# Attention, low-rank mixing and phase mixing on one core: the first batch's phases and weights in another order, Q and K in three buffers

## The chip, the cores and the metric

The kernel runs on one core of a Trainium2 chip. The metric is the device time of one launch in microseconds (us), the median of a few runs; lower is better.

## What is computed

The reference, cut to what matters. There are 4 batches, 8 heads, 768 tokens and a head size of 48, so a row has D = 384 features.

```python
mag = np.sqrt(a_re * a_re + a_im * a_im)
scale = np.minimum(mag, 0.999) / (mag + 1e-06)
a_re_n, a_im_n = (a_re * scale, a_im * scale)
for t in range(S):                       # the state is complex, k v^T is added to its real part
    new_re = ar * S_re - ai * S_im
    new_im = ar * S_im + ai * S_re
    S_re, S_im = (new_re + kv, new_im)
    y[:, :, t] = np.einsum('bhd,bhde->bhe', q[:, :, t], S_re)
# y as x of shape (batch, seq, 384)
h = xt @ U @ V                           # over the tokens, rank 32
u = x + h.transpose(0, 2, 1)
x = u + np.maximum(u @ w_ch1, 0.0) @ w_ch2
theta = x @ w_theta
y = np.einsum('ts,bsd->btd', w_tok_r, x * cos(theta)) + np.einsum('ts,bsd->btd', w_tok_i, x * sin(theta))
u = x + y
out = u + np.maximum(u @ w_ch, 0.0)
```

## The kernel before

The recurrence over tokens is done as chunked attention. A batch is C = 6 chunks of P = 128 tokens. For every token and feature the kernel takes the logarithm of the magnitude of `a` and its angle, sums both over the tokens (the sums of the angle, in turns, are the phases), and multiplies Q and K by a decay factor (`scaled`) and then by the sine and the cosine of the phase (`turned`, r = 0 and 1), which gives the tensor `QKz`. DMAs turn its features into rows (`to_rows`, two DMAs for each r, since features are spread over heads in a wide and a fine group). On these rows PE computes the scores of the chunk (`scores`), DVE masks them (`mask_scores`), and PE adds masked scores times V and Q times the state (`values`). The state goes from chunk to chunk: PE transposes K (`key_columns`), ACT copies it (`keys_to_sbuf`), PE multiplies K and V (`keys_values`), ACT copies the product (L735), PE transposes it (`turn_state`), and DVE adds and decays the state (`next_state`, L1085 to L1091). After the chunks come the low-rank mixing (`rank`, `u_rows`, `u_mixed`), the two channel products (`up`, `down`), `theta`, the token products (`mix`) and the last channel product (`channels`). Those products take their operands in two parts: a rounded part that ACT makes (`round_piece` for the weights, L867) and the rest, which POOL makes by subtraction (`split`, L534). Weights come in 15 pieces: 0 to 11 for the two channel products, 12 to 14 for the last two matrices.

Five programs, one an engine, run beside each other and meet in semaphores; what stands in a program is done in that order. The order is written out by hand. SP issues nearly all DMAs. From batch 1 on, the phases and decays of the next batch are computed during the channel products of the batch before. Batch 0 has its own way (functions named `first_...`): ACT and DVE make logarithms and tangents chunk by chunk, PE sums the decays (`first_sums`), ACT takes six arctangents (`first_angle`, L640), and PE sums the angles of a chunk over its tokens by a product with a triangular matrix and adds the carry of the chunk before (`first_turns`). A negative real part needs half a turn more; `phasor[:, c, 0, :]` holds 0 or 0.5 for that, and PE adds it with three products of its own, beside the three for the angle, which are multiplied by `tri_turn` (the triangle over pi). DVE then takes the carry of the chunk and the fraction of the phase (`first_phase`, L995 to L1006), ACT sine and cosine (`first_sin_cos`, L646 to L649).

In batch 0 the order around the change is: five phases on PE and DVE, then the scores of chunk 0, then phase 5 on PE (`first_turns(C - 1)` in `attention`) and on DVE behind the masks of chunk 0. Between phases DVE scales and turns Q and K of chunks 0 and 1. ACT issues the r = 1 half of chunk 0's rows itself (`first_rows`). ACT rounds two pieces behind each chunk of batch 0, POOL splits eight of them, then squares the next batch's `a`, and splits the last four among the work for batch 1. Q and K come through two buffers, `qk_in`, which are the first 4 D columns of `stream`; `load_qk(b, c)` waits until chunk c - 2 is turned. SP loads Q and K of chunk c + 3 and V of chunk c + 2 ahead of the rows of chunk c + 2.

## Time and profile before

| | |
|---|---|
| median of 3 runs | 774.71 us (773.43 to 777.81) |
| the profiled execution's own time | 773.47 us |
| its span, from the first to the last instruction | 771.7 us |
| PE, matmul | 731.8 us busy (95%) |
| DVE | 499.9 us busy (65%) |
| ACT | 403.8 us busy (52%) |
| POOL | 223.6 us busy (29%) |
| mean granted clock of PE | 0.989 of full speed |
| chain that ended last, by engine | PE 81%, DVE 7%, ACT 4%, DMA 4% |

Busy time is the union of an engine's instructions. In the span of batch 0 up to 98.6 us the chain goes through all engines; behind it PE is nearly always busy. A timeline row gives start and length in us, then how many instructions of one kind it stands for, and in brackets how long the engine was idle before it and what ended that.

### The profile page before, as it was taken

To read this page: it belongs to the slowest core of one execution; us is meant where nothing else is said; L and a number is where in the kernel's file an instruction comes from. 1 tells how busy PE (TensorE), PEld (TensorE's weight loads), DVE (VectorE), ACT (ScalarE), POOL (GpSimd) and SP (SyncE) were. 2 spreads that over 40 slices of the span, in tenths; PEclk is the share of its full clock that TensorE was granted. 3 is DMA by queue.
4 is the path that set the end of the run, shared out by engine and by line. 5 is a ranking of instruction groups with operands and counts; after the bars stand their busy time and mean duration, and the time that the engine had idled before them with its cause. 6 is when DMAs were issued, how large, how long until landed. Compare 5 with 4: busy or idle time off the path is not lost.

```text
span 771.7 us, 13433 instructions
## 1 busy us (share of the span) xinstructions
PE 731.8 (95%) x5118; PEld 704.2 (91%) x5118; DVE 499.9 (65%) x905; ACT 403.8 (52%) x875; POOL 223.6 (29%) x175
## 2 busy tenths in 40 slices
PE   3588999999999999999999999999999999999998
PEld 3578799999999879999999879999999979999998
DVE  7759488798468657696558758597448832224534
ACT  7847456755365447664464537574464621223531
POOL 0006663533520063323430053232530010113350
PEclk9889999999999999999999999999999999999999
DMA  9566620100257750010246860010136940000121
GB/s 301 169 184 180 196 87 1 41 1 2 82 145 213 209 174 1 4 39 1 62 133 184 218 205 21 2 42 1 50 96 185 254 135 23 2 1 0 42 62 62
DMA packets 42735, 73.48 MB, mean 95 GB/s; under 512 B 8784, under 2 KB 23376, under 8 KB 42672
## 3 DMA queue, kind: packets, MB, share of 16 engines
q1 hardware_dynamic: 42384, 72.23, 31.9%
q8 instruction: 41, 0.67, 0.4%
q10 hardware_dynamic: 288, 0.39, 0.2%
q14 instruction: 22, 0.18, 0.1%
HBM read 48.96 MB, written 4.72 MB: 70 GB/s over the span
## 4 chain that ended last, share of the span: by engine, by line
PE 81%; DVE 7%; ACT 4%; DMA 4%; issue 2%; SPq 1%; DVEq 0%; ACTq 0%
PE bank L1302 78%; DMA stream<-stream 2%; DMA region<-stream 1%; PE bank L1507 1%; DVE stream L1041 1%; DVE logr L915 1%; DVE logr L911 1%; PE bank L1418 1%; PE bank L1343 1%; PE bank L1375 1%; SPq L357 1%; DVE phasor L904 1%; DVE stream L1055 0%; SPq L358 0%; DVE ST L1072 0%
## 5 line engine op out<-in xcount | busy, mean ns | idle before, releaser
L1302 PE MATMUL bank<-uT,w_sb 128*128 128x384 f32 x864 | 166.5, 339 | 0.0
L1302 PE MATMUL bank<-hT,w_sb 128*128 128x384 f32 x864 | 165.0, 336 | 0.0
L1302 PE MATMUL bank<-tok,z 128*128 128x384 f32 x864 | 158.7, 337 | 0.6 <-issue 0.2
L1302 PEld LDWEIGHTS bank<-uT,w_sb 128*128 128x128 f32 x864 | 151.6, 190 | 1.8 <-ACT uT L756 1.2
L1302 PEld LDWEIGHTS bank<-hT,w_sb 128*128 128x128 f32 x864 | 151.1, 188 | 0.3 <-DVE hT L1200 0.3
L1302 PEld LDWEIGHTS bank<-tok,z 128*128 128x128 f32 x864 | 149.3, 188 | 1.7 <-POOL tok L539 1.7
L1200 DVE SCALAR_TENSOR_TENSOR hT<-bank,hT 128x384 fp32r<-128x384 f32 x96 | 52.8, 550 | 68.1 <-ACT hT L748 67.7
L748 ACT ACTIVATE hT<-bank 128x384 fp32r<-128x384 f32 x96 | 46.4, 484 | 75.4 <-PE bank L1302 75.3
L539 POOL TENSOR_TENSOR tok<-tok_low,tok 128x768 fp32r<-128x768 f32 x20 | 38.2, 1909 | 86.7 <-ACT tok L778 86.7
L547 POOL TENSOR_TENSOR x_sb<-uT 128x384 f32<-128x384 f32 x24 | 25.1, 1077 | 104.1 <-DVE uT L1194 71.1
L514 POOL TENSOR_TENSOR logr<-stream 128x384 f32<-128x384 f32 x18 | 15.1, 841 | 102.1 <-DMA stream<-in_a 102.1
L534 POOL TENSOR_TENSOR w_sb<-w_raw,w_sb 128x768 fp32r<-128x768 f32 x12 | 26.1, 2189 | 63.7 <-ACT w_sb L867 63.7
L553 POOL TENSOR_TENSOR xs<-x_sb,xs 128x384 fp32r<-128x384 f32 x24 | 27.7, 1173 | 54.5 <-ACT xs L765 54.5
L1302 PE MATMUL bank<-tc_sb,xs 128*128 128x384 f32 x216 | 41.4, 335 | 0.0
L1072 DVE TENSOR_TENSOR ST<-bank,tri 128x512 f32<-128x512 f32 x48 | 32.5, 687 | 13.2 <-PE bank L1302 12.9
L1302 PE MATMUL bank<-xs,tc_sb 128*128 128x384 f32 x216 | 38.9, 337 | 0.0
L519 POOL TENSOR_TENSOR phasor<-stream,phasor 128x384 f32<-128x384 f32 x18 | 18.8, 1046 | 68.6 <-ACT phasor L665 68.6
L1302 PEld LDWEIGHTS bank<-tc_sb,xs 128*128 128x128 f32 x216 | 37.9, 188 | 0.0
L1302 PEld LDWEIGHTS bank<-xs,tc_sb 128*128 128x128 f32 x216 | 37.4, 188 | 0.0
L539 POOL TENSOR_TENSOR tok<-scale,tok 128x768 fp32r<-128x768 f32 x16 | 29.4, 1848 | 25.9 <-ACT tok L778 25.9
L1302 PE MATMUL bank<-region 96*128 96x128 f32 x256 | 33.3, 286 | 3.6 <-DMA region<-stream 3.6
L1302 PEld LDWEIGHTS bank<-region 96*128 96x128 f32 x256 | 31.7, 200 | 4.1 <-DMA region<-stream 4.0
(183 smaller groups left out, 1309.5 us busy)
## 6 DMA issues: line engine op xcount, KB each, us to landing
stream<-in_qk SPq DMA_DIRECT2D x24, 384.0 KB, 3.9
tok_low<-in_w_tok SPq DMA_DIRECT2D x20, 384.0 KB, 3.5
stream<-in_a SPq DMA_DIRECT2D x19, 384.0 KB, 3.8
scale<-in_w_tok SPq DMA_DIRECT2D x16, 384.0 KB, 4.2
w_raw<-in_w SPq DMA_DIRECT2D x12, 384.0 KB, 7.8
region<-qk SPq DMA_DIRECT2D x16, 256.0 KB, 3.6
region<-stream SPq DMA_DIRECT2D x15, 256.0 KB, 3.2
stream<-in_v SPq DMA_DIRECT2D x16, 192.0 KB, 4.3
```

What stands on the lines that cost most here:

```text
L357: sp.dma_start(to[wide, :, :, :], QKz[c % 2][:, r, 0:2, :, :]).then_inc(s_rows_in[c % 3].sem, 16)
L514: ins = g.tensor_tensor(to, part, part, ALU.mult)
L519: g.tensor_tensor(phasor[:, c, 1, :], a_part(b, c, 1), phasor[:, c, 1, :], ALU.mult)\
L534: g.tensor_tensor(part[1], raw, part[0].bitcast(F32), ALU.subtract).then_inc(s_split.sem, 1)
L539: g.tensor_tensor(tok[:, m % 4, 1, :], tok_raw(m)[1], tok[:, m % 4, 0, :].bitcast(F32), ALU.subtract)\
L547: g.tensor_tensor(x_sb[:, n, :], uT[:, 0, kd, :].bitcast(F32), uT[:, 1, kd, :].bitcast(F32), ALU.add)\
L553: g.tensor_tensor(xs[0][:, 1, n % KD, :], x_sb[:, n, :], xs[0][:, 0, n % KD, :].bitcast(F32), ALU.subtract)\
L748: a.activation(hT[:, n % 3, 0, :], hidden_bank[n % 3][:, 0:N2], ACT.Relu).then_inc(s_hid_hi.sem, 1)
L904: d.tensor_tensor(mag, mag, qk[:, c * D:(c + 1) * D], ALU.add).then_inc(s_den.sem, 1)
L1072: d.tensor_tensor(ST[:, 4 * i:4 * i + 4, :], heads(score_bank[i][:, :]), tri[:, :].unsqueeze(1).broadcast_to([P, 4, P]), ALU.mult)\
L1200: d.scalar_tensor_tensor(hT[:, n % 3, 1, :], hidden_bank[n % 3][:, 0:N2], 0.0, hT[:, n % 3, 0, :].bitcast(F32), ALU.max, ALU.subtract)\
L1302: return t.matmul(o, lhsT, rhs, start=start, stop=stop, is_transpose=turned)
```

## The change

It has four parts.

1. Batch 0's sign term leaves PE. A new DVE operation a chunk (`first_turn`) multiplies the angle by 1/pi and adds the half turn, in place; `first_turns` on PE has three products with `tri` instead of six, and waits for that operation; `tri_turn` is gone.
2. All six phases stand ahead of the first scores, on PE and on DVE. `key_columns(0, 0)` comes after three phases, not four. V's split stands behind the phases; the scaling of chunk 1 behind phase 2.
3. Weight pieces 0 to 3 are rounded on ACT one by one between the first sines and cosines, 4 to 9 behind the sixth, 10 and 11 behind chunks 0 and 1. POOL splits all twelve in a row ahead of the next batch's squares. Pieces 12 to 14 are loaded during chunk 2. ACT issues its half of chunk 0's rows before the third sine, not after.
4. Q and K have a third buffer, `qk_third`; `load_qk(b, c)` waits for chunk c - 3. SP issues the rows of chunk c + 2 first, then Q and K of chunk c + 4, then V of chunk c + 2. Chunk 2 of the next batch is loaded in the middle of the batch before.

```diff
-        qk_in = [stream[:, at * D:(at + 2) * D].rearrange("p (i j t) -> p i j t", i=G, j=2) for at in (0, 2)]
+        qk_third = sb("qk_third", [P, 2 * D])
+        qk_in = [at.rearrange("p (i j t) -> p i j t", i=G, j=2)
+                 for at in (stream[:, 0:2 * D], stream[:, 2 * D:4 * D], qk_third[:, :])]
...
-        EARLY = 2 * PIECES - 4
+        EARLY = 2 * PIECES
...
             def load_qk(b, c):
-                if c >= 2:
-                    sp.wait_ge(s_Q.sem, s_Q.at(b, c - 1))
+                if c >= 3:
+                    sp.wait_ge(s_Q.sem, s_Q.at(b, c - 2))
...
                 for c in range(C - 1):
-                    if c + 3 < C and (c >= 1 or b == 0):
-                        load_qk(b, c + 3)
+                    if c + 2 < C:
+                        to_rows(b, c + 2)
+                    if c + 4 < C:
+                        load_qk(b, c + 4)
                     if c >= 1 and c + 2 < C:
                         load_v(b, c + 2)
-                    if c + 2 < C:
-                        to_rows(b, c + 2)
...
+                    if b == 0 and c == 2:
+                        for n in range(2 * PIECES, STAGED):
+                            load_piece(n)
...
                     sp.wait_ge(s_quot.sem, s_quot.at(b_next, C))
+                    load_qk(b_next, 2)
...
             to_rows(0, 0)
-            load_qk(0, 2)
             to_rows(0, 1)
+            load_qk(0, 3)
             gains_to_rows(0)
-            for n in range(2 * PIECES, STAGED):
-                load_piece(n)
...
-                    if b == 1 and c < 3:
-                        split(EARLY + 1 + c)
...
-                if b == 0:
-                    split(EARLY)
...
                     attention(b, c)
-                    if b == 0:
-                        round_piece(2 * c)
-                        round_piece(2 * c + 1)
+                    if b == 0 and c < 2:
+                        round_piece(2 * PIECES - 2 + c)
...
+            round_piece(0)
             for c in range(C):
+                if c == G - 1:
+                    first_rows()
                 if c == G:
-                    first_rows()
                     keys_to_sbuf(0, 0)
                 first_sin_cos(c)
+                if c < G:
+                    round_piece(c + 1)
+            for n in range(G + 1, 2 * PIECES - 2):
+                round_piece(n)
...
+            def first_turn(c):
+
+                angle_c = phasor[:, c, 1, :]
+                dve.wait_ge(s_atan.sem, c + 1)
+                d.scalar_tensor_tensor(angle_c, angle_c, 1 / math.pi, phasor[:, c, 0, :], ALU.mult, ALU.add)\
+                    .then_inc(s_first_turn.sem, 1)
...
-                    if b == c == 0:
-                        first_phase(C - 1)
...
             def first_turns(c):
-                pe.wait_ge(s_atan.sem, c + 1)
+                pe.wait_ge(s_first_turn.sem, c + 1)
...
-                    mm(to, phasor[:, c, 1, at], tri_turn[:, :], start=i == 0, stop=False)
-                    ins = mm(to, phasor[:, c, 0, at], tri[:, :], start=False, stop=c == 0 and i == G - 1)
+                    ins = mm(to, phasor[:, c, 1, at], tri[:, :], start=i == 0, stop=c == 0 and i == G - 1)
...
-                if b == c == 0:
-                    first_turns(C - 1)
...
-            for c in range(G + 1):
+            for c in range(G):
                 first_turns(c)
             key_columns(0, 0)
-            first_turns(G + 1)
+            for c in range(G, C):
+                first_turns(c)
```

**DVE, from the first scaling to the first masks.** L1041 (L1051 in the change) is `scaled`, L995 to L1006 (L1005 to L1016) a phase, L1055 (L1065) `turned`, L1172 and L1174 (L1180 and L1182) V's split, L1072 (L1082) the masks. Before, from the first products of chunk 0 on:

```order
L1055 TENSOR_TENSOR stream<-stream,phasor 128x768 x2
L995 COPY carry<-bank 128x3
L1004 TENSOR_SCALAR phasor<-bank 128x384
L1006 TENSOR_TENSOR phasor<-bank,phasor 128x384
L1055 TENSOR_TENSOR qk<-stream,phasor 128x768 x2
```

The change:

```order
L999 SCALAR_TENSOR_TENSOR phasor<-phasor 128x384 x2
L1065 TENSOR_TENSOR stream<-stream,phasor 128x768 x2
L1005 COPY carry<-bank 128x3
L1014 TENSOR_SCALAR phasor<-bank 128x384
L1016 TENSOR_TENSOR phasor<-bank,phasor 128x384
L1051 TENSOR_TENSOR stream<-stream,first_scale 128x768
L1005 COPY carry<-bank 128x3
L1014 TENSOR_SCALAR phasor<-bank 128x384
L1016 TENSOR_TENSOR phasor<-bank,phasor 128x384
L1065 TENSOR_TENSOR qk<-stream,phasor 128x768 x2
```

The last two of the six sign additions (L999) stand ahead of chunk 0's products, and the scaling of chunk 1 and one more phase between these and chunk 1's.

**ACT, from the arctangents to chunk 0.** L640 (L639) are the arctangents, the three lines from L646 (L645) a sine and cosine, L655 and L656 (L654 and L655) the DMAs of `first_rows`, L867 (L865) a rounding, L735 (L734) the copy of the K-V product. Before, around the sixth sine:

```order
L646 ACTIVATE phasor<-phasor 128x384
L648 ACTIVATE phasor<-phasor,half_pi 128x384
L649 ACTIVATE phasor<-phasor 128x384
L735 ACTIVATE tA<-bank 112x384
L742 ACTIVATE region<-bank 128x512
L867 ACTIVATE w_sb<-w_raw 128x768 x2
```

The change:

```order
L645 ACTIVATE phasor<-phasor 128x384
L647 ACTIVATE phasor<-phasor,half_pi 128x384
L648 ACTIVATE phasor<-phasor 128x384
L865 ACTIVATE w_sb<-w_raw 128x768 x6
L734 ACTIVATE tA<-bank 112x384
L741 ACTIVATE region<-bank 128x512
L865 ACTIVATE w_sb<-w_raw 128x768
```

Six roundings now stand between the sixth sine and the copy of the K-V product.

**SP, chunks 1 and 2 of batch 1.** L357 and L358 (L359 and L360) are `to_rows`, L334 (L336) `load_qk`, L341 (L343) `load_v`, L392 (L394) `store`. Before, from the end of chunk 3's rows to chunk 4's:

```order
L358 DMA region<-qk 16x8x256
L392 DMA out<-tB 128x384 [waits s_out]
L392 DMA out<-tC 128x384 [waits s_out]
L334 DMA stream<-in_qk 128x768 [waits s_Q]
L341 DMA stream<-in_v 128x384 [waits s_yt]
L357 DMA stream<-stream 32x4x512 [waits s_Q,s_yt]
```

The change:

```order
L360 DMA region<-qk 16x8x256
L336 DMA qk_third<-in_qk 128x768 [waits s_Q]
L343 DMA stream<-in_v 128x384 [waits s_yt]
L394 DMA out<-tB 128x384 [waits s_out]
L394 DMA out<-tC 128x384 [waits s_out]
L359 DMA stream<-stream 32x4x512 [waits s_Q,s_yt]
```

The V transfer in this piece is that of chunk 3 instead of chunk 4; chunk 4's now stands behind chunk 4's rows.

## Rows read from the trace of the kernel before

**Rows 1.** Windows: stretch, busy us (count) of PE, PEld, DVE, ACT, POOL; clock, DMA share, GB/s.

```profile
98.60:237.40 138.80, 137.79 (x793) 136.34 (x793) 105.20 (x186) 82.00 (x173) 58.12 (x42) 0.99 0.17 52
```

**Rows 2.** Timeline of PE, first batch: start, length, engine, line, operation, count [idle].

```profile
37.18 1.21 PE L1302 MATMUL bank<-carry,ident 128*128 128x128 f32 x6
...
48.57 3.78 PE L1302 MATMUL bank<-region 96*128 96x128 f32 x16 [3.27 <-DMA region<-stream]
```

**Rows 3.** Timeline of DVE, first batch, same columns.

```profile
34.87 0.16 DVE L995 COPY carry<-bank 128x3 f32<-128x3 f32 x1 [0.53 <-PE bank L1302]
...
35.52 0.56 DVE L1006 TENSOR_TENSOR phasor<-bank,phasor 128x384 f32<-128x384 f32 x1
...
39.56 1.81 DVE L1055 TENSOR_TENSOR stream<-stream,phasor 128x768 f32<-128x768 f32 x2
...
50.69 0.69 DVE L1072 TENSOR_TENSOR ST<-bank,tri 128x512 f32<-128x512 f32 x1 [4.13 <-PE bank L1302]
...
56.80 0.95 DVE L1041 TENSOR_TENSOR stream<-stream,first_scale 128x768 f32<-128x768 f32 x1
```

**Rows 4.** Timeline of ACT, first batch; ACTq is a DMA that ACT issues.

```profile
32.57 2.59 ACT L640 ACTIVATE phasor<-phasor 128x384 f32<-128x384 f32 x6
...
43.83 0.61 ACTq L656 DMA_DIRECT2D region<-stream  x1
...
58.41 0.47 ACT L735 ACTIVATE tA<-bank 112x384 f32<-112x384 f32 x1
...
59.25 1.57 ACT L867 ACTIVATE w_sb<-w_raw 128x768 fp32r<-128x768 f32 x2
```

**Rows 5.** Windows: the stretch of the first scores, columns as in rows 1.

```profile
48.50:52.20 3.70, 3.63 (x17) 3.63 (x18) 0.69 (x1) 0.15 (x1) 0.00 (x0) 0.50 0.69 149
```

**Rows 6.** Lengths (ns, min/median/max) of two lines, and timeline of POOL and DVE.

```profile
L534 POOL TENSOR_TENSOR w_sb<-w_raw,w_sb x12: 1812/2169/2772, 60.2 to 122.0; 128x768 fp32r<-128x768 f32 x12
...
L1091 DVE TENSOR_TENSOR state<-state_sum,gain_rows x20: 553/555/1604, 60.2 to 621.8; 96x384 f32<-96x384 f32 x20
...
66.38 2.21 POOL L534 TENSOR_TENSOR w_sb<-w_raw,w_sb 128x768 fp32r<-128x768 f32 x1 [2.15 <-ACT w_sb L867]
...
66.38 4.95 POOL L534 TENSOR_TENSOR w_sb<-w_raw,w_sb 128x768 fp32r<-128x768 f32 x2 [2.15 <-ACT w_sb L867]
...
65.09 1.83 DVE L1055 TENSOR_TENSOR qk<-stream,phasor 128x768 f32<-128x768 f32 x2
...
67.41 1.60 DVE L1091 TENSOR_TENSOR state<-state_sum,gain_rows 96x384 f32<-96x384 f32 x1
```

**Rows 7.** Timeline of POOL and DVE: three scans beside a square, and alone.

```profile
108.85 0.94 POOL L514 TENSOR_TENSOR logr<-stream 128x384 f32<-128x384 f32 x1
...
109.14 2.15 DVE L915 TENSOR_TENSOR_SCAN logr<-logr,qk 128x128 f32<-128x128 f32 x3
...
129.16 1.06 DVE L915 TENSOR_TENSOR_SCAN logr<-logr,qk 128x128 f32<-128x128 f32 x3
```

**Rows 8.** Timeline of DVE: masks of chunks 1 and 4, then two chunks of batch 1.

```profile
61.10 0.69 DVE L1072 TENSOR_TENSOR ST<-bank,tri 128x512 f32<-128x512 f32 x1 [0.34 <-PE bank L1302]
...
83.10 1.27 DVE L1072 TENSOR_TENSOR ST<-bank,tri 128x512 f32<-128x512 f32 x2
...
249.12 0.69 DVE L1072 TENSOR_TENSOR ST<-bank,tri 128x512 f32<-128x512 f32 x1 [0.16 <-PE bank L1302]
...
255.06 0.69 DVE L1072 TENSOR_TENSOR ST<-bank,tri 128x512 f32<-128x512 f32 x1 [0.23 <-PE bank L1302]
```

**Rows 9.** Timeline of PE in batches 1 and 2, and one window (DMA share second last).

```profile
260.76 2.05 PE L1302 MATMUL bank<-stream 96*128 96x128 f32 x16 [0.69 <-DMA stream<-stream]
...
425.49 2.05 PE L1302 MATMUL bank<-region 96*128 96x128 f32 x16 [0.33 <-DMA region<-stream]
...
438.67 2.05 PE L1302 MATMUL bank<-stream 96*128 96x128 f32 x16 [1.03 <-DMA stream<-stream]
...
250.00:252.00 2.00, 2.00 (x39) 1.86 (x39) 1.70 (x3) 1.70 (x5) 0.00 (x0) 1.00 1.10 220
```

39 lines of the change are left out of this document (22 added, 17 removed).

## The prediction

> **What bounds the kernel now.** I read the windows first. From 98.6 to 237.4 us PE is busy for 137.8 of 138.8 us [rows 1]: products of the first batch's second half and of the mixing leave nothing to win, and splits that run there on POOL cost nothing. What the change can touch is the first batch up to 98.6 us and the attention chunks of batches 1 to 3.
>
> The timelines of the first batch come next. PE waits 3.27 us for the turned rows of chunk 0 [rows 2]; after that it runs its first 16 score passes in 3.78 us, where the same 16 take 2.05 us later [rows 2, 9], because the granted clock stands at 0.50, the lower of its two levels, 1.2 GHz [rows 5]. Last comes phase 5, behind the scores on PE; DVE can scale Q and K of chunk 2 only at 56.80, and ACT copies the first K-V product only at 58.41 [rows 3, 4]. From then to the mask of chunk 4 the chunks follow in (83.10 - 61.10) / 3 = 7.3 us, where batch 1 needs 5.94 [rows 8]. The difference is POOL. A split has 1.81 us of its own, and DVE's state update, 0.55 of its own, took 1.60 while a split ran [rows 6]. The reader is to see that both never work at once if DVE reads two operands from SBUF. Nor does DVE keep its turn: three scans, 1.06 us alone, took 2.15 because POOL's second square went in between them [rows 7]. POOL's first split of the pair at 66.38 took 2.21, so it really began about 66.78, 0.14 before the end of the product that it met [rows 6].
>
> In batches 1 to 3 PE waits only for rows that DMA turns round: 0.69 us in batch 1 and again in batch 3, of which one row is shown, 1.03 in batch 2, and 0.33 at chunk 2 of batch 2; the DMA engines' busy share is 1.10 there [rows 9].
>
> **The change, part by part.** The sum goes against the profiled execution, 773.47 us (span 771.7, 1.8 around it); its difference is then put on the median, 774.71. About 0.5%, 3.9 us, is what a measurement can tell from no change.
>
> *Sign on DVE.* PE loses 3 of 6 products per phase; DVE gets six additions of 0.55 us (its 384-wide two-operand length [rows 3]). The first one stands on the path: PE starts 0.6 us later and needs some 0.7 less, so phase 0 ends where it did, at 35.9 or so (36.08 before). PE ran slowly then (three carries 1.21 us [rows 2]), so phase 1 ends near 38.3.
>
> *Rounding early.* Arctangents end at 35.16 [rows 4]. Rounding is 0.79 us a piece, a sine and cosine about 1.5 (three of ACT's 0.43 steps and its own wait [rows 4]). Pieces 0, 1, 2 are then rounded by 35.9, 38.3 and 40.6, and each starts a split of 1.8 us. The fifth sign addition starts at 38.2, the split goes in behind it, the sixth addition waits until 40.3, and the third split lands before or between the two products of chunk 0. These end near 44.2; without POOL 41.1, before 41.37 [rows 3]. ACT's half of the turned rows, issued at 43.83 before [rows 4], goes out at about 44.9 and lands near 48.2, helped by an emptier queue: no gain.
>
> *All phases first.* DVE: phase 2 to 45.3 (1.2 us a phase [rows 3]), scaling of chunk 1 to 46.2, phase 3, which needs PE's six transposes, its turns and its carries, to 47.6, the two products of chunk 1 with split 3 between them to 50.9, phase 4 to 52.1, PE's carries 1.2 more, phase 5 to 53.3, V's split, a cast of 0.55 and a 768-wide difference of 0.95, to 54.8. The two masks end near 56.5, so chunk 2 is scaled at the same time as before (56.80 [rows 3]). ACT ends its last sine at 54.9, then rounds six pieces, 4.7 us, and comes to the K-V copy at 59.6; before 58.41. So the named idle time is used, but it is not idle any more: the phases have taken PE's and DVE's.
>
> *Splits in the chunks.* Eight splits are still to come from 55.8 on, POOL having a backlog. A turn of a 768-wide operation and a split lasts 0.95 + 1.82 less two overlaps of 0.13, 2.51 us; with the state update 2.11. A chunk has three of the first and one of the second: 9.6 us. The mask of chunk 1 comes at 65.4, of chunk 2 at 75.0, and then, POOL being done, two steps of 5.94 bring that of chunk 4 to 86.9: 3.8 us later than before. This is the upper end. The lower: DVE keeps the port through neighbouring products, two holds a chunk as now. Then chunk 0's products end at 42.5, the mask of chunk 1 comes near 60.1, and 22.0 us later, at the old pace, chunk 4's at 82.1: 1.0 us earlier. The scans [rows 7] speak for the upper end. Against it stands POOL's second split of the pair at 66.38: the pair took 4.95, so the second began at about 69.5, when the state update, done at 69.01, and the first mask had both passed it [rows 6]. I take the middle, **+1.4 us**. That ACT no longer rounds two pieces just ahead of the last copy of x is worth **-0.1** at most, taken as that.
>
> The Trainium skill, SBUF — State Buffer, section "SBUF: two separate sides", calls the pair of ports that DVE and GpSimd share an exclusive lock held for a whole instruction, and puts GpSimd's release at DVE's end plus about 115 ns. The lock agrees with the 1.60 us; the delay does not agree with a start 0.14 us ahead of that end [rows 6]. By the page eight turns would be 0.25 us longer each, 2.0 us in all, and the sum 775.8 instead of 773.8.
>
> *Three buffers, rows first.* The same bytes go out between the turned rows of chunk 3 and those of chunk 4, except V of chunk 4, 192 KB, which now follows: at 220 GB/s [rows 9] 0.85 us. Of the waits 0.69, 1.03 and 0.69 this takes 0.69, 0.85, 0.69, **-2.2 us**; the 0.33 stays. Bounds 0 (the total queue is as full) and -2.7 (all of them). V of chunk 4 must then land within the 7 us or so until PE's K-V products of that chunk; if this cover is gone, they wait. In the first batch the three last weight pieces now go out ahead of chunk 5's rows instead of beside the first ones: 1.15 MB, up to 1 us, within the range.
>
> *Splits taken out of the second half:* nothing, PE covers them [rows 1].
>
> Sum: 774.71 + 1.4 - 0.1 - 2.2 = **773.8 us**, no change that can be told.
>
> **Rivals.**
> - *DVE keeps its turn* (lower end above, -1.0, and all of -2.3): 771.4. For it: the passing over at 68 us. Against: the scans.
> - *POOL never meets DVE on the path.* DVE waited 4.13 us before the first mask [rows 3], so holds may fall there. Without any, chunk 0's products end at 41.1, chunk 2 is scaled at 51.4, the K-V copy comes at 55.3, the mask of chunk 1 at 58.0, that of chunk 4 at 58.0 + 3 x 5.94 = 75.8, 7.3 earlier: 774.71 - 7.3 - 2.3 = 765.1. Against it stands that ACT releases splits exactly while DVE has its two-operand work.
> - *Slower: the clock falls again.* With 9.6 us chunks PE, which has 5.94 of work, waits 3.6 us for the masks of chunks 1 and 2. The one wait of 3.27 us before the first scores was followed by 0.50 for 3.7 us [rows 2, 5], which costs half of that, 1.85. It decides once a wait reaches about that length. Two such and the upper end: 774.71 + 3.8 + 3.7 - 2.3 = 779.9.
> - *The reordering does nothing:* the engines stay full and the waits stay: 776.0.
> - *POOL gets the port later than I read*, which is what the page's figure above would mean: 775.8, worked out from eight turns of 0.25 us.
>
> **How the numbers follow.** Forecast 0.42; DVE keeps its turn 0.20; no holds on the path 0.16; clock falls 0.12; reordering does nothing 0.06; later port 0.04. Faster by over 0.5% (below 770.8): all of the third case, half of the second, a little of the first, 0.30. Slower (above 778.6): 0.12. The rest 0.58. The range goes from 766.0, which leaves out the better half of the third case, to 779.0, which leaves out the worse half of the fourth.
>
> **What would show it.** In the profile of the changed kernel: the first splits start at 36 us and the sixth sign addition or the first product of Q lasts 2 us or more; chunk 0's products end at 43.5 to 44.5; the K-V copy on ACT comes later than 58.4; in the next two chunks the products of Q are stretched to more than 2 us each, and the chunks last over 8 us; chunks 3 and 4 come at the pace of 5.9; PE's waits for turned rows in batches 1 to 3 shrink to about 0.5 us in all; the 98.6 to 237.4 us stretch keeps its length of 138.8. Wrong would be: products of Q at their own 0.95 us throughout (third case), a clock below 1 in the chunks (fourth), or the masks of chunk 4 earlier than 80 us.

## The result and the profile after

The changed kernel takes 780.55 us, the median of 14 runs (777.71 to 783.18), against 773.61 for the kernel before in the same session: a ratio of 1.0081 (95% 1.0066 to 1.0096), so it is slower by 0.8%. Its profiled execution took 781.37 us with a span of 779.6. In the code of after the masks are L1082 (L1072 before), the scaling L1051, the products L1065, the state update L1101, PE's products L1317 (L1302), a split L535 (L534), a rounding L865 (L867) and the copy of the K-V product L734 (L735); other kernels differ from these by a few lines. A product here is DVE's turning of Q and K, L1065, and a hold is the time that a DVE operation waits for a split that is under way.

First the timeline of DVE in the first batch, columns as in [rows 2].

```profile
37.00 1.71 DVE L999 SCALAR_TENSOR_TENSOR phasor<-phasor 128x384 f32<-128x384 f32 x1
...
39.75 2.45 DVE L999 SCALAR_TENSOR_TENSOR phasor<-phasor 128x384 f32<-128x384 f32 x2
42.12 3.42 DVE L1065 TENSOR_TENSOR stream<-stream,phasor 128x768 f32<-128x768 f32 x2
...
50.24 2.61 DVE L1065 TENSOR_TENSOR qk<-stream,phasor 128x768 f32<-128x768 f32 x2
...
56.64 1.29 DVE L1082 TENSOR_TENSOR ST<-bank,tri 128x512 f32<-128x512 f32 x2
...
57.85 0.95 DVE L1051 TENSOR_TENSOR qk_third<-qk_third,first_scale 128x768 f32<-128x768 f32 x1
...
58.83 2.45 DVE L1065 TENSOR_TENSOR stream<-qk_third,phasor 128x768 f32<-128x768 f32 x1
...
64.34 1.52 DVE L1101 TENSOR_TENSOR state<-state_sum,gain_rows 96x384 f32<-96x384 f32 x1
65.90 0.69 DVE L1082 TENSOR_TENSOR ST<-bank,tri 128x512 f32<-128x512 f32 x1
...
67.83 2.31 DVE L1051 TENSOR_TENSOR stream<-stream,first_scale 128x768 f32<-128x768 f32 x1
70.17 4.96 DVE L1065 TENSOR_TENSOR qk<-stream,phasor 128x768 f32<-128x768 f32 x2
...
77.13 1.27 DVE L1082 TENSOR_TENSOR ST<-bank,tri 128x512 f32<-128x512 f32 x2
```

A fourth sign addition of 1.71 us in place of 0.55, a pair of products of 3.42 in place of 1.81 [rows 3], a pair of 4.96: every DVE operation with two operands in SBUF that meets a split under way waits for it. The first masks, at 50.69 before [rows 3], come at 56.64; those of chunk 1, at 61.10 [rows 8], at 65.90; those of chunk 2 at 77.13, where the kernel before had them at 68.9.

POOL in the same stretch. The first row is the first of the four splits ahead of the scores. The last row is all eight splits that stand in a row behind them, the three ahead of it the first of these, the second with the third, and the third with the fourth, so that they start at 57.88, 60.43 and 62.92:

```profile
36.48 1.81 POOL L535 TENSOR_TENSOR w_sb<-w_raw,w_sb 128x768 fp32r<-128x768 f32 x1 [34.10 <-ACT w_sb L865]
...
57.88 2.59 POOL L535 TENSOR_TENSOR w_sb<-w_raw,w_sb 128x768 fp32r<-128x768 f32 x1 [6.71 <-ACT w_sb L865]
...
60.43 5.02 POOL L535 TENSOR_TENSOR w_sb<-w_raw,w_sb 128x768 fp32r<-128x768 f32 x2
...
62.92 4.62 POOL L535 TENSOR_TENSOR w_sb<-w_raw,w_sb 128x768 fp32r<-128x768 f32 x2
...
57.88 18.92 POOL L535 TENSOR_TENSOR w_sb<-w_raw,w_sb 128x768 fp32r<-128x768 f32 x8 [6.71 <-ACT w_sb L865]
```

ACT behind its last sine, and PE, where the bracket says how long it was idle and for what:

```profile
56.97 4.49 ACT L865 ACTIVATE w_sb<-w_raw 128x768 fp32r<-128x768 f32 x6
61.37 0.47 ACT L734 ACTIVATE tA<-bank 112x384 f32<-112x384 f32 x1
```

```profile
53.74 1.95 PE L1317 MATMUL bank<-region 96*128 96x128 f32 x16
...
61.89 0.98 PE L1389 MATMUL bank<-ident,tA 112*96 112x112 f32 x4 [3.26 <-ACT tA L734]
...
77.95 0.67 PE L1317 MATMUL bank<-ST,tD 128*48 128x128 f32 x4 [3.65 <-DVE ST L1082]
```

The copy of the K-V sums stands behind six roundings and comes at 61.37 (58.41 before [rows 4]); PE waits 3.26 us for it and 3.65 us for the masks of chunk 2. Windows of PE around these two waits (the clock is third from the end):

```profile
60.00:64.00 4.00, 2.11 (x11) 2.11 (x12) 4.00 (x3) 3.50 (x7) 4.00 (x3) 0.50 0.34 98
...
68.00:74.00 6.00, 6.00 (x86) 5.67 (x82) 5.97 (x3) 3.60 (x9) 6.00 (x3) 1.00 0.07 26
...
80.00:86.00 6.00, 6.00 (x48) 5.49 (x46) 3.29 (x6) 1.98 (x5) 0.00 (x0) 0.69 0.78 199
```

Each wait is followed by a stretch at 1.2 GHz; the last window, 0.69, holds a part of the second one. What went well shows too: the first 16 score passes took 1.95 us at the full clock, where they took 3.78 before [rows 2]. A phase's products now stand right ahead of them, in place of the wait of 3.27 us.

Where the 7.9 us between the two profiled spans lie: the channel products of batch 0 start at 107.1 in place of 98.6 us, which is 8.5; the attention of batches 1 to 3, from first mask to channel products, gives back 0.47 and 0.88 and loses 0.41; the rest of the layers gives 2.6 back in batch 0 and loses 1.6 and 1.4 in batches 1 and 2. Pieces of that last size come and go between profiles of kernels with the same work there, as the section on the hardware tells, so they are not put down to the change. The waits of PE for turned rows in batches 1 to 3 [rows 9] are down to 0.2 us, but PE now waits for V, here in batch 2, and 1.3 us in batch 3:

```profile
435.33 0.87 PE L1317 MATMUL bank<-qk,tD 128*48 128x96 f32 x16 [0.99 <-DMA tD<-in_v]
```

### The profile page after: what moved, and what is told of

Same layout as the page of the kernel before. It is cut to its first block, busy times and chain, and to the rows that moved or that the text cites. A ratio compares the mean times of both kernels' runs of the same rounds, so it can differ in the third digit from the quotient of the medians.

```text
span 779.6 us, 13366 instructions
## 1 busy us (share of the span) xinstructions
PE 735.4 (94%) x5082; PEld 708.3 (91%) x5082; DVE 505.7 (65%) x910; ACT 405.0 (52%) x875; POOL 224.6 (29%) x175
## 4 chain that ended last, share of the span: by engine, by line
PE 87%; DVE 5%; ACT 3%; DMA 3%; issue 1%; SPq 1%; DVEq 0%
PE bank L1317 82%; DMA tD<-in_v 2%; PE bank L1357 1%; PE bank L1519 1%; PE bank L1389 1%; PE bank L1430 1%; DVE stream L1065 1%; DVE qk L1065 1%; DVE phasor L999 1%; DMA region<-stream 1%; ACT w_sb L865 1%; SPq L359 0%; ACT first_scale L631 0%; DVE Z L1189 0%; DMA stream<-in_a 0%
## 5 line engine op out<-in xcount | busy, mean ns | idle before, releaser
L1317 PE MATMUL bank<-uT,w_sb 128*128 128x384 f32 x864 | 167.9, 342 | 0.0
L1317 PE MATMUL bank<-hT,w_sb 128*128 128x384 f32 x864 | 165.0, 336 | 0.0
L1317 PE MATMUL bank<-tok,z 128*128 128x384 f32 x864 | 158.7, 337 | 0.6 <-issue 0.3
L1317 PEld LDWEIGHTS bank<-uT,w_sb 128*128 128x128 f32 x864 | 153.1, 191 | 1.7 <-ACT uT L755 1.2
L1317 PEld LDWEIGHTS bank<-hT,w_sb 128*128 128x128 f32 x864 | 151.1, 188 | 0.3 <-DVE hT L1208 0.3
L1317 PEld LDWEIGHTS bank<-tok,z 128*128 128x128 f32 x864 | 149.3, 188 | 1.8 <-POOL tok L540 1.8
L747 ACT ACTIVATE hT<-bank 128x384 fp32r<-128x384 f32 x96 | 46.5, 484 | 85.5 <-PE bank L1317 85.3
L1317 PE MATMUL bank<-tc_sb,xs 128*128 128x384 f32 x216 | 41.4, 335 | 0.0
L535 POOL TENSOR_TENSOR w_sb<-w_raw,w_sb 128x768 fp32r<-128x768 f32 x12 | 26.8, 2257 | 47.6 <-ACT w_sb L865 47.6
L1317 PE MATMUL bank<-xs,tc_sb 128*128 128x384 f32 x216 | 38.8, 337 | 0.0
L1082 DVE TENSOR_TENSOR ST<-bank,tri 128x512 f32<-128x512 f32 x48 | 32.6, 688 | 8.9 <-PE bank L1317 8.5
L1317 PEld LDWEIGHTS bank<-tc_sb,xs 128*128 128x128 f32 x216 | 37.9, 188 | 0.0
L1317 PEld LDWEIGHTS bank<-xs,tc_sb 128*128 128x128 f32 x216 | 37.4, 188 | 0.0
L741 ACT ACTIVATE region<-bank 128x512 f32<-128x512 f32 x24 | 14.3, 596 | 42.2 <-PE bank L1317 42.2
L709 ACT ACTIVATE qk<-bank 128x256 f32<-128x256 f32 x40 | 21.5, 538 | 22.9 <-PE bank L1357 22.9
```

The lines of the kernel that those rows point to most:

```text
L535: g.tensor_tensor(part[1], raw, part[0].bitcast(F32), ALU.subtract).then_inc(s_split.sem, 1)
L709: a.activation(Kn[:, :, to_wide].rearrange("p (h i) d -> p h i d", i=2), wide, ACT.Copy)
L747: a.activation(hT[:, n % 3, 0, :], hidden_bank[n % 3][:, 0:N2], ACT.Relu).then_inc(s_hid_hi.sem, 1)
L1082: d.tensor_tensor(ST[:, 4 * i:4 * i + 4, :], heads(score_bank[i][:, :]), tri[:, :].unsqueeze(1).broadcast_to([P, 4, P]), ALU.mult)\
L1317: return t.matmul(o, lhsT, rhs, start=start, stop=stop, is_transpose=turned)
```

## The experiments

Ratios are to the kernel before, run beside each of them, with a 95% interval, from 5 to 14 runs each. The trace says where batch 0 stands, in us: the first masks of its six chunks, and the start of its channel products ("end").

| kernel | median us | ratio | masks of batch 0 | end |
|---|---|---|---|---|
| before | 773.6 to 775.0 | 1 | 50.7 61.1 68.9 76.0 83.1 87.5 | 98.6 |
| changed | 780.55 | 1.0081 (1.0066 to 1.0096) | 56.6 65.9 77.1 84.7 90.7 96.1 | 107.1 |
| e1_gated | 775.86 | 1.0003 (0.9980 to 1.0027) | 51.2 60.4 67.1 73.1 79.7 86.9 | 99.2 |
| e2_early_splits | 781.58 | 1.0070 (1.0047 to 1.0094) | 51.7 68.4 78.3 84.8 90.7 96.2 | 107.2 |
| e3_buffers | 773.29 | 0.9975 (0.9951 to 0.9999) | 52.1 62.7 70.5 77.6 84.7 89.1 | 100.2 |
| e4_late_rounds | 769.71 | 0.9934 (0.9911 to 0.9957) | 51.0 57.1 64.3 71.4 78.5 82.9 | 94.0 |
| e5_sign | 774.76 | 1.0007 (0.9988 to 1.0027) | 52.7 62.3 70.1 77.2 84.3 88.7 | 99.8 |
| e6_ahead | 768.68 | 0.9928 (0.9904 to 0.9952) | 51.2 57.2 64.4 71.5 78.6 83.0 | 94.1 |
| e7_v_first | 767.88 | 0.9912 (0.9893 to 0.9930) | 52.0 58.1 65.3 72.3 79.4 83.8 | 94.9 |
| e8_gated_late | 768.94 | 0.9930 (0.9906 to 0.9954) | 49.5 54.5 59.6 65.7 72.3 78.0 | 88.5 |
| e9_copy_first | 773.58 | 0.9993 (0.9975 to 1.0011) | 51.7 56.8 67.2 73.1 79.8 85.4 | 95.6 |
| e10_half_splits | 782.97 | 1.0108 (1.0075 to 1.0142) | 56.8 66.0 73.6 80.3 85.3 95.6 | 107.9 |
| e11_best_half | 767.63 | 0.9909 (0.9886 to 0.9931) | 51.2 56.4 63.1 69.8 76.5 83.2 | 94.4 |
| e12_four_held | 780.89 | 1.0094 (1.0067 to 1.0120) | 56.8 66.0 72.6 78.5 85.1 93.4 | 106.7 |
| e13_after_spread | 772.69 | 0.9974 (0.9950 to 0.9997) | 56.4 62.4 69.6 76.7 83.8 88.2 | 99.2 |
| e14_half_pieces | 764.89 | 0.9867 (0.9830 to 0.9903) | 51.7 56.9 63.6 70.3 77.0 81.4 | 92.5 |

The places in the table carry a difference between profiles that lies ahead of phase 0: DVE ends phase 0 at 36.1 us in the kernel before, 37.1 in the changed kernel, and at 35.7 to 38.3 in the others, kernels with the same code up to there among them. Counted from there, the first mask comes after 13.96 us in e4, e6, e7, e9 and e14 alike, and after 19.56 in the changed kernel and e12, so that the four early splits cost 5.6 us there. Only e1 stands apart from its kind, with 15.30: PE ran slowly in its phase 2 (six passes in 1.49 us, in e9, with the same code, 0.83).

### Holds taken away, and each part alone

**e1_gated**: the changed kernel, POOL's early splits kept until DVE's last product of batch 0 (the gate), and the last four of the twelve back among the work for batch 1.

```diff
                 if b == 0:
+                    pool.wait_ge(s_Q.sem, s_Q.at(0, C))
                     for n in range(EARLY):
                         split(n)
```

> The changed kernel, ACT's early roundings kept, but POOL begins its splits only when DVE has turned Q and K of the last chunk of batch 0 (the last four splits stand where they stood before). Theory H (the splits hold the port that DVE's two-operand work needs, and that lost the time): products of Q at 0.95 us throughout, chunk 0's products done at about 41.5 instead of 45.5, masks of chunks 1 to 4 a pace of 5.9 to 6.5 us apart, first channel product before 98 instead of at 107.1, total 766 to 771. Theory K (the six roundings ahead of ACT's copy of the K-V product lost it): mask of chunk 1 still after 64, total 776 or more. Theory P (the phases ahead of the scores lost it): first scores no earlier than 52 and total 775 or more.

It came back to the time of before, the first mask at 51.2. Taking the holds away is thus worth 0.8% (give or take 0.3), and the 766 to 771 of theory H was too much. Batch 0 ended no earlier than before: the six roundings still stood ahead of the copy, with a wait of 3.3 us on PE, and PE waited for the rows of chunk 5, which SP issues behind three weight pieces. ACT and PE of e1:

```profile
51.52 4.49 ACT L870 ACTIVATE w_sb<-w_raw 128x768 fp32r<-128x768 f32 x6
55.92 0.47 ACT L739 ACTIVATE tA<-bank 112x384 f32<-112x384 f32 x1
```

```profile
85.22 3.10 PE L1322 MATMUL bank<-region 96*128 96x128 f32 x15 [1.84 <-DMA region<-qk]
```

**e2_early_splits**: the kernel before with the early roundings and splits alone.

```diff
+            round_piece(0)
             for c in range(C):
...
+                if c < G:
+                    round_piece(c + 1)
+            for n in range(G + 1, 2 * PIECES - 2):
+                round_piece(n)
```

> The kernel before with nothing but the early roundings and the twelve splits in a row. H: the whole loss is here and more: two or more holds among the products of chunks 0 and 1, mask of chunk 4 at 90 or later against 83.1, total 779 to 785. K: the copy of the K-V product at about 62 and the loss there, but the chunks after it at 7 us each: total 777 to 780. P: no loss, total 773 to 774.

This part alone costs 0.70%, where the changed kernel as a whole loses 0.81% and its other parts gain 0.66% (e4, below): the parts do not add up, since in the changed kernel this one costs 1.5% (changed against e4). The traces show one reason. The four early splits cost the first mask nothing here: it stands 14.1 us behind phase 0, in the kernel before 14.6, because DVE still had idle time ahead of the masks, 2.5 us of the 4.1 before [rows 3]. With all phases ahead of the scores the same four cost 5.6 us. What e2 loses it loses later: with phase 5 still behind the scores, the six roundings start at 59.44 and PE waits 6 us for the copy. PE's waits in e2 from 50 to 108 us (total, times, longest):

```profile
PE bank L1375 <- ACT tA L731: 6.0, 1, 6.0
PE bank L1302 <- DVE ST L1072: 2.0, 1, 2.0
```

**e3_buffers**: the kernel before with the third buffer and rows first alone.

```diff
+                    if c + 2 < C:
+                        to_rows(b, c + 2)
-                    if c + 3 < C and (c >= 1 or b == 0):
-                        load_qk(b, c + 3)
+                    if c + 4 < C:
+                        load_qk(b, c + 4)
```

> The kernel before with nothing but the third Q and K buffer and the rows issued ahead of the loads. All theories: batch 0 unchanged within 1 us. In batches 1 to 3 PE's waits for turned rows (2.7 us in all before) fall under 1 us; the changed kernel's trace showed instead waits of 1.0 and 1.3 us for V of chunk 5. If these belong to the new order, they are here too, total -1.0 to +0.5 us; if they came from elsewhere, total -2.5 us.

A gain of 1.9 us (0.1 to 3.8), and of the waits in [rows 9] 0.2 us are left. The expectation names V of chunk 5; the wait in the changed kernel stands in the third chunk's work of the batch, so it is V of chunk 2, which goes to the same buffer.

**e4_late_rounds**: the changed kernel with roundings and splits back where they were: two roundings behind each chunk, eight splits early, four among the work for batch 1.

```diff
-                    if b == 0 and c < 2:
-                        round_piece(2 * PIECES - 2 + c)
+                    if b == 0:
+                        round_piece(2 * c)
+                        round_piece(2 * c + 1)
```

> The changed kernel with roundings and splits put back behind the chunks, two and two. H: chunk 0's products done at about 41.5, mask of chunk 1 at 56 to 58, then 7 us a chunk as before, total 767 to 772. K: about the same. P: the loss stays, total 777 or more.

Faster than before by 0.66%: the rest of the change is a gain. DVE reaches the second masks at 57.1 in place of 61.1, and PE has no longer wait than 1.0 us from the first masks to the channel products.

### Which part brings that gain

**e5_sign**: the kernel before with `first_turn` on DVE and three products a phase on PE, nothing else (the diff is part 1 of the change).

> The kernel before with the sign term added on DVE and nothing else. What e4_late_rounds gained on the kernel before (0.66%) lies either in this or in the phases put ahead of the first scores (or in the buffers). If the sign term on its own carries it, this run comes out 4 to 5 us faster, about 770. If it only trades 18 matmuls for six DVE operations of 0.5 us ahead of the same chain (phase 0 began 34.9 us before and 35.9 us in e4, phase 1 at 38.4 us in both), it is within 1 us of before, 774 to 776, and the first mask stands at 50.5 to 51.5 us.

No gain: 1.0007. Its first masks, at 52.7, come 1.2 us later than I had put them, but phase 0 ended 2.2 us later than before: counted from there they come after 14.4 us, before after 14.6. Here the sign additions stand behind V's split and the scaling of chunk 1; how much of the 2.2 us that is, and how much lies between profiles, is not shown.

**e6_ahead**: e4 with two buffers and SP's old order.

```diff
-                    if c + 2 < C:
-                        to_rows(b, c + 2)
-                    if c + 4 < C:
-                        load_qk(b, c + 4)
+                    if c + 3 < C and (c >= 1 or b == 0):
+                        load_qk(b, c + 3)
```

> e4_late_rounds without the third Q and K buffer and with rows behind the loads as before: so the kernel before plus the sign term and all six phases ahead of the first scores. If the last phase (which in the kernel before stands behind chunk 0's scores, its matmuls first at 55.7 us, and holds back the K-V copy at 58.4 us) was the cost, the second mask is at 57 us in place of 61.1, all of batch 0 ends 4 us earlier and the run takes 770 to 771.5. If the gain of e4 came from the buffers, it is about 774 to 775.

All of it: 0.9928. The first masks come no earlier, the second ones 6.0 us behind them in place of 10.4. So the gain is phase 5 ahead of the first scores: ACT copies the K-V product at 51.49 (58.41 before), and DVE scales chunk 2 at 52.36 (56.80 before). The smaller moves that e6 also has (the three weight pieces behind later rows, `first_rows` before the third sine) were not run alone. On top of it the buffers and the new order of SP add nothing that shows (e4 against e6, 0.9934 to 0.9928).

**e7_v_first**: why the buffers add nothing. In batches 1 to 3 the new order puts a 384 KB load of Q and K ahead of V of chunk 2. SP's issues in e4, and what PE waited for:

```profile
416.19 0.60 SPq L336 DMA_DIRECT2D stream<-in_qk  x1
416.84 0.46 SPq L343 DMA_DIRECT2D tD<-in_v  x1
```

```profile
423.89 0.87 PE L1317 MATMUL bank<-qk,tD 128*48 128x96 f32 x16 [1.96 <-DMA tD<-in_v]
```

```diff
+                    if b and c == 0:
+                        sp.wait_ge(s_stored[2 * KD - 1].sem, s_stored[2 * KD - 1].at(b, 0))
+                        load_v(b, 2)
                     if c + 4 < C:
                         load_qk(b, c + 4)
...
-                    if b and c == 0:
-                        sp.wait_ge(s_stored[2 * KD - 1].sem, s_stored[2 * KD - 1].at(b, 0))
-                        load_v(b, 2)
```

> e4_late_rounds with one change in SP's order: in chunk 0 of batches 1 to 3 the load of V for chunk 2 is issued ahead of the 384 KB load of Q and K for chunk 4, and not behind it. In e4 PE waited 2.0 us in batch 2 and 1.4 us in batch 3 for this V. If the order in the queue makes it late, both waits go, the fourth mask follows the third after 5.9 us in every batch, and the run takes 766 to 768. If the transfer is slow because much else moves at that time, the waits stay above 1 us and the run takes 769 to 770.

The wait for V is gone, and waits of 1.1 and 0.3 us for rows stand in its place in batches 2 and 3. The ratio of 0.9912 lies within e4's interval: a gain is not shown. Why e3 has neither wait, with the same order, stays open, and so it is not shown either that this V is what took the buffers' gain.

### The splits later, one behind the other, or smaller

**e8_gated_late**: e7 with the gate of e1 and the weight pieces behind the rows of chunk 5.

```diff
+                    pool.wait_ge(s_Q.sem, s_Q.at(0, C))
...
-                    if b == 0 and c == 2:
+                    if b == 0 and c == 3:
```

> e7_v_first with GpSimd's first eight splits kept until DVE has done all its products of batch 0, and the last weight pieces issued behind the rows of chunk 5; the roundings on ACT stay two behind each chunk. If the pace of 7.1 us per chunk in batch 0 of the kernel before and of e4 is DVE held by the splits, four chunks now take 5.9 to 6.0 us each, batch 0 ends 4 to 5 us earlier and the run takes 761 to 764. If the pace is set by something else (ACT's two roundings of 0.8 us per chunk, or rows by DMA), it stays over 6.5 us, and the run takes 765 to 768. If the splits that now come late keep PE waiting for weights at the start of the layer behind, that shows as PE waits on L537 and takes back what was won.

Batch 0 ends at 88.5, 6.4 us ahead of e7, of which 2.4 lie ahead of phase 0 and say nothing. The first chunks follow at 5.1, 5.1 and 6.1 us, and DVE's operations keep their own lengths as long as no split runs: the pace of 7.1 us a chunk is DVE held by splits. But the run is no faster (761 to 764 was expected). From there to the first mask of batch 1 it takes 143.8 us, e7 139.2. POOL's squares for batch 1 start at 85.6 in e7 and 85.0 in e8, 9 us ahead of the channel products in e7 and 3.5 ahead of them in e8, so all that POOL, DVE and ACT prepare for batch 1 falls later into them; PE waits 3.8 us there for DVE (2.6 in e7), with a slow clock in the first window. That this is the cause is read from the trace; no run isolates it. Two windows of e8:

```profile
88.00:98.00 10.00, 8.92 (x39) 8.23 (x40) 9.22 (x8) 3.54 (x8) 8.05 (x9) 0.83 0.21 79
...
128.00:148.00 20.00, 17.81 (x104) 17.50 (x103) 14.64 (x29) 15.14 (x30) 10.48 (x8) 1.00 0.13 42
```

**e9_copy_first**: e1 with the six roundings behind ACT's work of chunk 0.

```diff
+                    if b == 0 and c == 0:
+                        for n in range(G + 1, 2 * PIECES - 2):
+                            round_piece(n)
...
-            for n in range(G + 1, 2 * PIECES - 2):
-                round_piece(n)
```

> e1_gated with one change on ACT: the six roundings that stood in a row ahead of the copy of chunk 0's K-V sums are issued behind ACT's work of chunk 0. In e1 that copy ended at 56.4 us (51.8 in e4), PE waited 3.3 us for it and then ran at half clock for about 5 us, and the second mask stood at 60.5 us. If the row of roundings is what delays it, the copy comes at about 51.5, the second mask at 54.5 to 55.5 and the run takes 769 to 771 (part of it comes back in the layer behind, as in e8). If the copy waits for something else, the second mask stays at 60 and the run at 775 to 776.

The copy came in time and the second mask at 56.8, but the row now stood ahead of the key copies of chunk 1 (ACT, first two rows), and PE waited 3.73 us there, with a slow clock behind. The profile names no releaser for that wait; it ended as the last of these copies did. The time is that of e1, not the 769 to 771 expected. A row of roundings costs in both places; two at a time (e4) show no such wait.

```profile
54.26 5.23 ACT L873 ACTIVATE w_sb<-w_raw 128x768 fp32r<-128x768 f32 x7
59.40 0.50 ACT L714 ACTIVATE qk<-bank 128x256 f32<-128x256 f32 x1
```

```profile
60.80 1.50 PE L1323 MATMUL bank<-qk,stream 128*48 128x96 f32 x16 [3.73 <-issue]
```

**e10_half_splits**: the changed kernel, each split in two halves.

```diff
+                for i in range(2):
+                    cut = (slice(None), slice(i * C * P // 2, (i + 1) * C * P // 2)) if n in up_pieces else (slice(None), i)
+                    ins = g.tensor_tensor(part[1][cut], raw[cut], part[0].bitcast(F32)[cut], ALU.subtract)
+                ins.then_inc(s_split.sem, 1)
```

> The changed kernel, where GpSimd makes each of its twelve early splits in two halves of 384 columns: the same elements in 24 instructions of about 1 us in place of 12 of 1.8. Nothing else. Theory of turns: when both engines have work queued, GpSimd and DVE take the shared side one instruction at a time each, so DVE pays one split for each of its own SBUF operations; halves make each payment about 1.0 in place of 1.8 us (though more of DVE's operations meet one). Then chunk 0's products end near 43 us in place of 45.5, the first mask is at 53.5 to 54.5 in place of 56.6, and the run takes 775 to 778. Rival, a split holds DVE for as long as GpSimd has work: the totals are the same and the run takes 780 to 782 with the first mask at 56 to 57.

DVE, POOL and PE of e10:

```profile
42.23 3.43 DVE L1071 TENSOR_TENSOR stream<-stream,phasor 128x768 f32<-128x768 f32 x2
...
58.97 3.31 DVE L1071 TENSOR_TENSOR stream<-qk_third,phasor 128x768 f32<-128x768 f32 x2
```

```profile
58.02 1.77 POOL L540 TENSOR_TENSOR w_sb<-w_raw,w_sb 128x384 fp32r<-128x384 f32 x1 [5.85 <-ACT w_sb L871]
...
58.02 23.25 POOL L540 TENSOR_TENSOR w_sb<-w_raw,w_sb 128x384 fp32r<-128x384 f32 x16 [5.85 <-ACT w_sb L871]
```

```profile
93.91 3.40 PE L1323 MATMUL bank<-region 96*128 96x128 f32 x16 [4.32 <-DMA region<-qk]
```

In the chunks the theory of turns holds: a pair of products takes 3.31 us in place of 4.94, and the halves beside it follow at 1.7 us. A rival by which a split holds DVE as long as POOL has work is out. Ahead of the first scores I was wrong: there each half met another DVE operation, the pair took 3.43 as before, and the first mask stayed at 56.8. The time, 775 to 778 expected, is no better either (1.0108 against 1.0081): PE waited 4.32 us for chunk 5's rows, and ran slowly behind.

**e11_best_half**: e7 with the same halves.

> e7_v_first, the fastest version so far (0.991 of before), with the same halves for the splits. In e7 two splits behind each chunk hold DVE's operations and the chunks of batch 0 take 7.1 us each, against 5.9 in the later batches. By the theory of turns half of that 1.2 us goes, the pace is 6.4 to 6.8, and the run takes 765 to 767. If four halves meet four of DVE's operations and cost as much as two whole ones, it stays at 7.1 and 767.5 to 768.5.

The pace fell from 7.1 to 6.7 us a chunk, but the time is that of e7, for PE now waited 2.22 us for the rows of chunk 5:

```profile
82.00 2.05 PE L1323 MATMUL bank<-region 96*128 96x128 f32 x16 [2.22 <-DMA region<-qk]
```

**e12_four_held**: e1 with the gate only behind the fourth split.

```diff
                     for n in range(EARLY):
+                        if n == 4:
+                            pool.wait_ge(s_Q.sem, s_Q.at(0, C))
                         split(n)
```

> e1_gated with the first four splits let go at once, as in the changed kernel, and the other four early ones kept until DVE has done its products of batch 0. It sizes the holds ahead of the first scores alone. By the traces of the changed kernel and e1 these cost 5.4 us on the first mask (56.6 against 51.2): the first mask is at 56 to 57 us and the run takes 780 to 782, so that the holds in chunks 1 and 2 would have cost the changed kernel little in the end. If slack behind the first scores takes some of it up, the first mask is still at 56 to 57, but the run takes 777 to 779.

The first four splits put 5.6 us on the first mask (against e9 too, counted from phase 0) and 0.9% on the time of e1, as expected (780 to 782). So e12, where no split meets DVE between the first masks and DVE's last product of batch 0, is no faster than the changed kernel (1.0094 against 1.0081). Its trace says where the two differ. A pair of products in e12, and PE's two longest waits:

```profile
69.11 1.83 DVE L1071 TENSOR_TENSOR qk<-stream,phasor 128x768 f32<-128x768 f32 x2
```

```profile
PE bank L1395 <- ACT tA L740: 3.3, 1, 3.3
PE bank L1323 <- DMA region<-qk: 2.4, 1, 2.4
```

The second masks come 9.3 us behind the first in both kernels: the copy behind six roundings sets that step, and the holds hide in it. The third masks follow after 6.5 us in e12 and after 11.2 in the changed kernel, whose fifth masks then stand 5.6 us later (90.7 and 85.1). e12 loses that again behind them: it waits for chunk 5's rows, and its channel products start 21.7 us behind the fifth masks, in the changed kernel 16.4.

**e13_after_spread**: the changed kernel with eight roundings two behind each chunk; the splits follow freely.

```diff
-                    if b == 0 and c < 2:
-                        round_piece(2 * PIECES - 2 + c)
+                    if b == 0 and c < 4:
+                        round_piece(G + 1 + 2 * c)
+                        round_piece(G + 2 + 2 * c)
...
-            for n in range(G + 1, 2 * PIECES - 2):
-                round_piece(n)
```

> The changed kernel with one change on ACT: the first four roundings stay in its idle time ahead of the first scores, and the other eight stand two behind each of the chunks 0 to 3, in place of six in a row ahead of the copy of the K-V sums. The splits follow without a gate. So the four holds ahead of the first scores stay (first mask at 56.6), and what goes is the wait for the K-V copy (3.3 us of PE, with the clock fall behind it) and the row of eight splits. If the holds ahead of the first scores cost 5 to 6 us to the end, the chunks behind follow at 7.1 us, attention of batch 0 ends near 99.5 and the run takes 774.5 to 776.5. If those first holds are the whole loss, it takes 779 to 781.

With the four early holds in it (first masks at 56.40) it is faster than the kernel before, by 0.26%, and 2 us faster than I had expected. DVE of e13, from the first masks to the second in 6.0 us, in the changed kernel 9.3:

```profile
56.40 1.29 DVE L1081 TENSOR_TENSOR ST<-bank,tri 128x512 f32<-128x512 f32 x2
...
62.44 1.27 DVE L1081 TENSOR_TENSOR ST<-bank,tri 128x512 f32<-128x512 f32 x2
```

**e14_half_pieces**: e11 with the weight pieces behind the rows of chunk 5 (`c == 3` for `c == 2`, as in e8).

> e11_best_half with the last three weight pieces issued behind the rows of chunk 5 in place of ahead of them. In e11 PE waited 2.2 us for those rows in batch 0 (1.8 in e1, 2.4 in e12, 4.3 in e10). If the order in the queue makes them late, the wait goes, the sixth mask follows the fifth after 5.5 us or less, and the run takes 765 to 766.5. If the layer behind, which waits for the squares of batch 1 and its weights, takes it back, it stays at 767 to 768.

The wait is gone (the sixth mask 4.4 us behind the fifth, in e11 6.7), and this version is the fastest: 0.9867 of before, 10 us. Its gain on e11, 0.4%, is at the edge of what the two intervals show.

### The sum

Taking 774.6 us for before, the ratios give: all phases ahead, -5.6 (e6); three buffers and rows first on top, +0.5, nothing that shows (e4 against e6); four splits ahead of the first scores, +3.1 (e13 against e4, give or take 2.5); six roundings in a row ahead of the copy, and eight splits in a row behind it, +8.3 (changed against e13, give or take 2.1). These are steps from one kernel to the next, so that they must add up to the +6.3, or 0.81%, measured; the sizes are worth no more than their intervals. For the four early splits e12 against e1 gives 7.0, give or take 2.7, instead of 3.1; the 5.6 us of the traces lies in both intervals.

The traces size the same steps at the fifth mask, counted from the end of phase 0: 47.0 us before, 41.4 in e4, 46.9 in e13, 53.6 in the changed kernel, so -5.7, +5.6 and +6.7. How the last step divides between the roundings and the splits in a row is shown in the trace alone, by e12 above; in the whole time no run shows it, since what the gate saves there comes back as other waits.

## Why the prediction was wrong

It gave 773.8 us, 766 to 779, with 0.12 for slower; the time is 780.55. The step that failed is the term for splits in the chunks, +1.4, and with it the clock, which was left out of the sum: together they measured +7.6 at the fifth mask. Point by point:

- **Sign on DVE**, no cost, phase 0 done at 35.9: it was done at 37.08 in this profile and at 35.90 in that of e1, whose DVE has the same work up to there, so this difference is one between profiles; e5 shows no cost. Right.
- **Rounding early.** Splits began at 36.48, 39.51 and 42.26, and chunk 0's products ended at 45.5, where the walk had 44.2; it had started 1.2 us too early with phase 0, and from there it held. Right, with the rest of the walk: the holds ahead of the first masks are in it.
- **All phases first.** The first masks were walked to about 56.5 and came at 56.64. The copy was walked to 59.6 and came at 61.37: the last sine had to stand behind that of phase 4, and ended at 57.07 in place of 54.9. That the 3.78 us of slow scores became 1.95 I had not counted.
- **Splits in the chunks: the step that failed.** The upper end, strict turns of 2.51 us, is what happened: the trace has 2.49 from one split to the next while DVE has products. I took the middle, +1.4, between it and a case in which DVE keeps its turn, so 28.0 us from the first masks to the fifth; strict turns alone gave 30.4, and 34.1 were measured. The row set against them, POOL's second split at 69.5 [rows 6], was read as DVE passing over POOL. The kernel before has the same once more, in the pair at 73.17, whose second split began at 76.6, and not in the last pair, where it began at 83.04, right at the end of the state update:

```profile
73.17 5.23 POOL L534 TENSOR_TENSOR w_sb<-w_raw,w_sb 128x768 fp32r<-128x768 f32 x2 [1.85 <-ACT w_sb L867]
...
82.73 2.13 POOL L534 TENSOR_TENSOR w_sb<-w_raw,w_sb 128x768 fp32r<-128x768 f32 x1
```

  In the changed kernel, where eight splits wait at once, no DVE operation of this kind passed. When POOL is passed over stays open.
- **The clock.** I kept two waits of 3.6 us with a slow clock behind each as a rival of its own at 0.12, and left it out of the sum. Yet the upper end's own chunks of 9.6 us against 5.94 of work on PE make that wait, so the two belong together. Measured are waits of 3.26 and 3.65 us, at 1.2 GHz behind each. The fifth mask came at 90.7, 7.6 later than before, where the upper end without the clock gave 86.9, or 3.8. The term of +1.4 thus measured +7.6, or 6.6 counted from the end of phase 0. The first of the two waits had another cause than I gave: not a mask but the copy behind six roundings, a wait that the walk contained (58.41 to 59.6) and priced only as lateness; by e12 it sets the second masks. The slow PE behind it also brought DVE's second mask of chunk 1 late (67.22), which is why the next step took 11.2 us and not 9.6. That the rival's 779.9 lies near the time is in part luck: it counts -2.3 for the buffers, which did not come.
- **ACT's last copy**, -0.1: too small to be tested.
- **Three buffers, rows first**, -2.2. On the kernel before it was right (e3, -1.9). In the changed kernel attention of batches 1 to 3 gained 0.9 in all, and e4 against e6 shows nothing. I named V of chunk 4 as what would be late next; late was V of chunk 2, behind the load of Q and K for chunk 4. The three weight pieces ahead of chunk 5's rows, put "within the range", make no wait here, where the chunks are slow; in e1, e10, e11 and e12 PE waits 1.8 to 4.3 us for those rows, and with the pieces behind them (e14 against e11) the wait is gone.
- **Splits taken out of the second half**, nothing: e8 shows that this place is not as free as [rows 1] made it look, since by its trace work that comes there late stops PE.
- The Trainium skill, SBUF — State Buffer, section "SBUF: two separate sides", says that whoever starts first has the shared pair for the whole instruction. The halves of e10 agree: a hold is as long as the other's instruction, and a turn takes 2.49 or 1.7 us. Its figure of about 115 ns behind DVE's end, which the page has from a DMA whose descriptors GpSimd writes, does not carry over to a split: in the changed kernel DVE's scaling ended at 58.80, and the first split's 2.59 us less its own 1.82 put its true start at 58.65. Turns were 2.49 us, not 0.25 longer, so the rival at 775.8 is out.

## What to carry to other kernels

An engine's idle time is not free if the work put there releases another engine that shares something with the critical one: here ACT's idle time was real, and its roundings let POOL loose on DVE. Two parts of a change can meet: the early splits cost the first mask nothing while DVE had slack there, and 5.6 us once the other part had used it up. When both sides have a queue, charge one full instruction of the other for each one of yours, not an average, and let them come a few at a time. Halving them brought the pace from 7.1 to 6.7 us a chunk, and no time until the rows behind came earlier too. Then carry each wait of PE that such a walk yields into the clock, and look at what stands behind the copy that PE waits for: a row of six short jobs there makes a wait of 3.3 us or more, and the same six in pairs make none.

## What the runs showed of the hardware

- Waits of 3.3 to 3.7 us on PE were each followed by a stretch at 1.2 GHz, by the granted clock in the windows above. For shorter ones the length of the wait alone does not tell: behind 2.22 us (e11) 16 score passes took 2.05 us, behind 1.84 us (e1) 15 of them took 3.10, and behind 1.64 us (e2) the first 16 took 3.78.
- Behind the attention of a batch PE has a few idle gaps, and in some batches of nearly every kernel a stretch of channel products then runs at half clock. It comes and goes between batches that do the same work. First the kernel before in batches 0 and 1, then the changed kernel in the same two:

```profile
98.00:120.00 22.00, 21.94 (x116) 21.50 (x117) 18.56 (x32) 12.27 (x28) 14.22 (x13) 0.92 0.16 58
...
278.00:300.00 22.00, 21.98 (x126) 21.54 (x127) 18.77 (x40) 15.31 (x35) 11.79 (x12) 1.00 0.16 56
```

```profile
106.00:128.00 22.00, 21.84 (x122) 21.14 (x123) 18.82 (x40) 15.24 (x35) 11.74 (x12) 1.00 0.18 66
...
283.00:305.00 22.00, 21.79 (x115) 21.30 (x115) 17.73 (x38) 15.44 (x34) 11.75 (x12) 0.92 0.17 59
```

  A clock of 0.92 over 22 us is some 3.5 us at the half clock, worth half of that or more in the length of that stage (first mask of the next batch less start of the channel products), which comes out at 137.2 to 140.3 us in all kernels but e8. Differences of that size between two single profiles say nothing of an edit; the medians have to.
- GpSimd and DVE take turns, instruction by instruction, when both have work queued: splits with DVE's scaling or products between them follow at 2.49 to 2.55 us, and in halves at 1.7 us. DVE's operations with an operand in PSUM kept their 0.54 to 0.69 us beside running splits, and where DVE had only such work (65.9 to 67.8 in the changed kernel) the splits followed each other at about their own 1.82 us. The turns are not without exception: besides the two splits in the kernel before, one half in e10, on record from 74.54, began its own work only at 75.65, at the end of a scaling that had passed it.
